# One kernel of attention, experts and gated product: loads, splits and joins around the scan put in other places

## The reference

```python
# 1: a recurrence with complex diagonal decay, gates limited to |a| <= 0.999
for t in range(S):
    new_re = ar * S_re - ai * S_im
    new_im = ar * S_im + ai * S_re
    S_re, S_im = (new_re + kv, new_im)          # kv = outer(k[t], v[t])
    y[:, :, t] = einsum('bhd,bhde->bhe', q[:, :, t], S_re)
# 2: top-1 experts, x = y as (3072, 384)
logits = x @ w_gate + modality_bias[modality_id]
out[mask] = gate_w[mask, None] * (relu(x[mask] @ w1[e]) @ w2[e])
# 3
out = ((x @ mid_w1) * (x @ mid_w2)) @ w3 @ w_out
```

## Time and profile before

| | us |
|---|---|
| median of 3 runs (lowest, highest) | 949.64 (948.28, 953.0) |
| the profiled execution, and its span | 949.64, 947.9 |
| PE busy in it | 798.0 (84%) |
| DVE, ACT, POOL busy | 510.3, 344.2, 128.1 |
| chain that ended last: PE, DVE | 69%, 19% |
| mean granted clock of PE, of full speed | 0.959 |

### The profile page before, as it was taken

How to read it: one execution, slowest core, us unless ns; L and a number is a source line. 1 busy time by engine, 2 the same in 40 slices (tenths; PEclk the granted TensorE clock), 3 DMA queues, 4 the chain that set the end, 5 groups by cost and what they waited for, 6 DMA issues and landing times.

```text
span 947.9 us, 11977 instructions
## 1 busy us (share of the span) xinstructions
PE 798.0 (84%) x4598; PEld 663.3 (70%) x4598; DVE 510.3 (54%) x980; ACT 344.2 (36%) x684; POOL 128.1 (14%) x127
## 2 busy tenths in 40 slices
PE   0039800699999998999999999999999999999995
PEld 0025400388888888778888888878989888888885
DVE  4999999999898855835445445452111121202010
ACT  6921201355545335345245335342222222213120
POOL 0201100000000322200000000002223232323231
PEclk9999955799999998999999999999999999999998
DMA  9981121557666675163433342233000000000000
GB/s 382 378 274 53 59 75 27 142 142 189 173 175 173 174 196 199 52 200 105 132 120 111 104 146 88 67 78 126 25 9 17 17 9 26 9 26 1 34 0 34
DMA packets 49014, 102.95 MB, mean 109 GB/s; under 512 B 12080, under 2 KB 31792, under 8 KB 46640
## 3 DMA queue, kind: packets, MB, share of 16 engines
q1 hardware_dynamic: 43312, 83.11, 28.5%
q0 software_dynamic: 5632, 18.94, 5.7%
HBM read 64.06 MB, written 18.95 MB: 88 GB/s over the span
## 4 chain that ended last, share of the span: by engine, by line
PE 69%; DVE 19%; DMA 3%; SPq 3%; ACT 3%; issue 2%; POOL 0%; DVEq 0%
PE moe_bank L515 18%; PE moe_bank L517 18%; PE moe_bank L516 18%; PE bank L1291 4%; DVE rows L1002 3%; DVE rows L1003 3%; PE bank L1325 2%; DVE gates L1005 2%; PE bank L1341 2%; PE bank L1257 2%; DVE gates L978 2%; DVE gates L1006 2%; SPq L670 1%; DMA gates<-a_im 1%; PE bank L1345 1%
## 5 line engine op out<-in xcount | busy, mean ns | idle before, releaser
L1835 DVE TENSOR_TENSOR u_sb<-x_in,moe_bank 128x512 f32<-128x512 f32 x48 | 33.0, 688 | 229.3 <-PE moe_bank L517 229.3
L1692 POOL TENSOR_TENSOR hid_lo<-u_sb,hid_hi 128x512 fp32r<-128x512 f32 x48 | 62.4, 1300 | 387.8 <-ACT hid_hi L1741 387.8
L517 PE MATMUL moe_bank<-xT_hi,w_lo 128*128 128x512 f32 x288 | 114.1, 396 | 0.0
L515 PE MATMUL moe_bank<-xT_hi,w_hi 128*128 128x512 f32 x288 | 113.7, 395 | 0.0
L516 PE MATMUL moe_bank<-xT_lo,w_hi 128*128 128x512 f32 x288 | 113.3, 394 | 0.0
L1270 PE MATMUL bank<-early_w_out,early_w3T 128*128 128x384 f32 x128 | 45.4, 511 | 66.0 <-DMA early_w_out<-w_out 62.6
L1270 PEld LDWEIGHTS bank<-early_w_out,early_w3T 128*128 128x128 f32 x128 | 24.8, 199 | 85.9 <-issue 64.7
L1756 ACT COPY x_in<-moe_bank 128x512 f32<-128x512 f32 x48 | 28.2, 587 | 149.8 <-PE moe_bank L517 149.8
L515 PE MATMUL moe_bank<-hid_hi,w_hi 128*128 128x512 f32 x168 | 68.0, 405 | 3.9 <-DVE hid_lo L510 2.0
L517 PE MATMUL moe_bank<-hid_hi,w_lo 128*128 128x512 f32 x168 | 67.1, 400 | 0.0
L516 PE MATMUL moe_bank<-hid_lo,w_hi 128*128 128x512 f32 x168 | 67.1, 400 | 0.0
(11 more groups left out here) (196 smaller groups left out, 1698.6 us busy)
## 6 DMA issues: line engine op xcount, KB each, us to landing
stage<-w SPq DMA_DIRECT2D x12, 1536.0 KB, 7.9
ks<-mags SPq DMA_DIRECT2D x48, 144.0 KB, 2.8
x_sorted<-early_zero POOLq DMA_DIRECT2D x8, 772.0 KB, 20.8
qs<-gates SPq DMA_DIRECT2D x40, 146.2 KB
x_in<-x_sorted SPq DMA_DIRECT2D x28, 193.0 KB, 3.7
gates<-a_re SPq DMA_DIRECT2D x4, 1170.0 KB, 12.3
gates<-a_im SPq DMA_DIRECT2D x4, 1170.0 KB, 14.6
spare<-k SPq DMA_DIRECT2D x4, 1152.0 KB, 5.5
```

The costliest lines, as they stand in the source:

```text
L515: nc.tensor.matmul(out, l_hi, r_hi, start=first, stop=False)
L517: return nc.tensor.matmul(out, l_lo, r_hi, start=False, stop=last)
L1692: nc.gpsimd.tensor_tensor(hid_lo[:, f], u_sb[:, f % 2], hid_hi[:, f].bitcast(F32), ALU.subtract).then_inc(u_lo_ready, 1)
L1835: nc.vector.tensor_tensor(u_sb[:, f % 2], a_sb[:, f % 2], bank_b[f % 2][:, :], ALU.mult).then_inc(u_ready, 1)
```

## The change

On SP, the wait for `first_ready` and the two value loads go to the last batch's turn, ahead of `stack_k(3, 1)`, and a W1 piece is issued behind each head's descriptors in it; W2 and x stay where they were. On ACT, W1's splits go from slots 7 and 8 to slots 5, 6 and 7, the scaling of `x_in` comes over from DVE (slots 7, 8, 9), three of W2's splits go into the eight hidden tiles, and the squares of stage 2 go from slot 0 to slot 1 of batch 0. On DVE, `finish(1, 3)` is done before the scan, `join(2, 2)` in slot 0 and `norm(2)` in slot 2; the low halves of W1 and W2 have other slots, W2's tiles 4 to 7 are subtracted by GpSimd behind its last scatter, and the table's parts stand one hidden tile earlier. In step 1 of the experts W1 is split ahead of x, as in the later steps. One wait in the general version is left out.

```diff
--- before.py
+++ after.py
@@ -643,13 +643,13 @@
         n_qs = n_ks + 1
         n_early = 2 * sum(g < -(-HU * D // P) for i in range(HU) for d, n, g, lane in pieces(HU + i))
         RANKS_AFTER = {5 * NCH - 1: 0, 6 * NCH - 1: 1, 7 * NCH - 1: 2}
-        EARLY_W1_HI = {7: (0, 1, 2, 3), 8: (4, 5, 6, 7)}
-        EARLY_W2_HI = {9: (0, 1, 2), 10: (3, 4, 5), 11: (6,)}
-        EARLY_X = {8: (0, 1), 9: (2, 3)}
-        BETWEEN_W1_LO = {8: 0, 9: 3, 10: 6}
-        EARLY_W1_LO = {8: (1, 2), 9: (4, 5), 10: (7,)}
-        BETWEEN_W2_LO = {11: 2}
-        EARLY_W2_LO = {10: (0, 1), 11: (3, 4)}
+        EARLY_W1_HI = {5: (0, 1, 2), 6: (3, 4, 5), 7: (6, 7)}
+        EARLY_W2_HI = {9: (0, 1), 10: (2, 3, 4)}
+        EARLY_X = {7: (0,), 8: (1, 2), 9: (3,)}
+        EARLY_W1_LO = {6: (0, 1), 8: (4, 5), 9: (7,)}
+        EARLY_W2_LO = {10: (1, 2)}
+        BETWEEN_W1_LO = {7: 2, 8: 3, 9: 6}
+        BETWEEN_W2_LO = {10: 0, 11: 3}
...
             return gates[:, x, b * GB:(b + 1) * GB].rearrange("p g (c t) -> p (g c) t", t=PITCH)[:, :, 0:CH]
...
 
-            def stack_k(b, m, planes=((0, seeds), (1, norms))):
+            def stack_k(b, m, first=None, planes=((0, seeds), (1, norms))):
                 for i in range(HU):
                     for d, n, g, lane in pieces(HU * m + i):
                         for c, plane_of in planes:
                             rows = slice(c * D + d, c * D + d + n)
                             sp.dma_start(ks[m][rows, i], plane_of[b][lane:lane + n, g * NCH:(g + 1) * NCH].rearrange(
                                 "p c t -> p (c t)")).then_inc(ks_in[m], DMA)
+                    if first is not None:
+                        load_w1(first, i)
...
                 cols = slice(i * (F // HU), (i + 1) * (F // HU))
...
             stack_q(sp, 0, 1, (RE, IM), range(G1))
             sp.wait_ge(k_half_ready, 1)
-            stack_k(0, 0, ((0, seeds),))
+            stack_k(0, 0, None, ((0, seeds),))
             sp.wait_ge(kt_ready, 1)
-            stack_k(0, 0, ((1, norms),))
+            stack_k(0, 0, None, ((1, norms),))
+            e = None
             for b in range(B):
                 sp.wait_ge(kinv_ready, 2 * b + 2)
                 if b + 1 < B:
                     load_k(b + 1)
                 if b:
                     sp.wait_ge(yT_psum, b * SLOTS)
+                if b == B - 1:
+                    sp.wait_ge(R.first_ready, 1)
+                    e = sp.value_load(L.table[0:1, L.FIRST:L.FIRST + 1], min_val=0, max_val=E - 1)
+                    row = sp.value_load(L.table[0:1, L.ROW0:L.ROW0 + 1], min_val=0, max_val=E * N - BLOCK)
                 sp.wait_ge(kt_ready, 2 * b + 2)
-                stack_k(b, 1)
+                stack_k(b, 1, e)
                 if b:
                     load_v(b, 1)
                 sp.wait_ge(ks_in[1], (b + 1) * (DMA * n_ks))
@@ -754,12 +761,7 @@
                     sp.wait_ge(ks_in[0], (b + 2) * (DMA * n_ks))
                     sp.wait_ge(qt_ready, 2 * b + 2)
                     stack_q(sp, b + 1, 0)
-            sp.wait_ge(R.first_ready, 1)
-            e = sp.value_load(L.table[0:1, L.FIRST:L.FIRST + 1], min_val=0, max_val=E - 1)
-            row = sp.value_load(L.table[0:1, L.ROW0:L.ROW0 + 1], min_val=0, max_val=E * N - BLOCK)
             sp.wait_ge(qs_in[1], B * (DMA * n_qs))
-            for i in range(HU):
-                load_w1(e, i)
             for i in range(HU // 2):
...
             sp.wait_ge(R.sorted_early, L.groups[1][1] * DMA)
@@ -854,7 +856,7 @@
 
...
 
-                if b == 0 and slot == 0:
+                if b == 0 and slot == 1:
                     squares_of(2)
                 if b + 1 < B:
                     if slot == (2 if b == 0 else 1):
@@ -874,13 +876,15 @@
                 if b == B - 1:
                     if slot == 4:
                         route_exp(nc, act, L, R, b - 1)
-                    if slot == 7:
+                    if slot == 5:
                         act.wait_ge(W.w1_first, HU * DMA)
                         act.wait_ge(qt_ready, 2 * B - 1)
                         for i in range(NU):
                             act.wait_ge(ks_in[i], B * (DMA * n_ks))
                     for f in EARLY_W1_HI.get(slot, ()):
                         split_w1_hi(nc, L, L.stage1, f, W.w1_hi_ready)
+                    for q in EARLY_X.get(slot, ()):
+                        scale_x(nc, act, L, W, 0, q)
                     if slot == 9:
                         act.wait_ge(W.w2_first, HU * DMA)
                     for f in EARLY_W2_HI.get(slot, ()):
@@ -928,8 +932,8 @@
             route_exp(nc, act, L, R, B)
             for f in range(KF):
                 hidden_high(nc, act, L, W, bank_scores[f % 2][:, :], 0, f)
-                if f == 0:
-                    split_w2_hi(nc, L, KF - 1, W.w2_hi_ready)
+                if 1 <= f <= 3:
+                    split_w2_hi(nc, L, f + 4, W.w2_hi_ready)
...
             nc.gpsimd.memset(shift[:, 0:1], MAG_EPS)
@@ -952,6 +956,10 @@
                     for loaded in W.x_loaded:
                         pool.wait_ge(loaded, DMA)
                 route_scatter(nc, pool, L, io, R, r)
+            for f in range(4, KF):
+                pool.wait_ge(W.w2_hi_ready, f + 1)
+                nc.gpsimd.tensor_tensor(L.w2_lo[:, f], L.stage2[:, f], L.w2_hi[:, f].bitcast(F32),
+                                        ALU.subtract).then_inc(W.w2_lo_ready, 1)
 
...
             def im_square(b):
@@ -1091,25 +1099,23 @@
                 finish(0, step)
             norm(1)
             join(2, 0)
-            for step in range(3):
+            for step in range(4):
                 finish(1, step)
-            for step in (1, 2):
-                join(2, step)
+            join(2, 1)
 
             def prepare(b, slot):
 
                 now, first, second, after = 2 * b + 1, 2 * b + 2, 2 * b + 3, 2 * b + 4
                 if slot == 0:
-                    if b == 0:
-                        finish(now, 3)
                     finish(now, 4)
                 elif slot == 1:
                     finish(now, 5)
                     finish(now, 6)
                 if b == 0:
-                    if slot == 1:
+                    if slot == 0:
+                        join(first, 2)
+                    elif slot == 2:
                         norm(first)
-                    elif slot == 2:
                         join(second, 0)
                     elif slot == 3:
                         join(second, 1)
@@ -1170,10 +1176,6 @@
                     elif slot == 11:
                         for k in range(2):
                             x_low(nc, dve, L, W, first_xT[k][:, :], 0, k)
-                    for q in EARLY_X.get(slot, ()):
-                        dve.wait_ge(W.x_loaded[q], DMA)
-                        nc.vector.tensor_scalar(L.x_in[:, q, 0:DM], L.x_in[:, q, 0:DM], L.x_in[:, q, DM + 1:DM + 2], None,
-                                                ALU.mult).then_inc(W.x_scaled, 1)
                     for f in EARLY_W1_LO.get(slot, ()):
                         split_w1_lo(nc, dve, L, L.stage1, f, W.w1_hi_ready, f + 1, W.w1_lo_ready)
                     for f in EARLY_W2_LO.get(slot, ()):
@@ -1226,13 +1228,10 @@
             first_low(1)
             V.read_rank(B, last_rank, True)
             V.place(B)
-            for f in (5, 6):
-                split_w2_lo(nc, dve, L, f, W.w2_hi_ready, f + 1, W.w2_lo_ready)
+            V.table_blocks()
             first_low(2)
-            V.table_blocks()
-            split_w2_lo(nc, dve, L, KF - 1, W.w2_hi_ready, KF, W.w2_lo_ready)
+            V.table_steps()
             first_low(3)
-            V.table_steps()
             V.table_pick(slice(0, 2))
             first_low(4)
             V.table_pick(slice(2, 4))
@@ -1550,7 +1549,6 @@
                 V.table_pick(slice(0, 4))
                 V.table_rows()
                 V.table_store()
-                wait_sorted(dve, L, A)
...
             with pe.If(general(pe)):
@@ -1717,12 +1715,9 @@
             def step(j):
                 for q in range(BT):
                     scale_x(nc, act, L, W, j, q)
-                if j > 1:
-                    w1_highs(w1_in, j, w1_hi_ready)
+                w1_highs(w1_in, j, w1_hi_ready)
                 for k in range(KD):
                     x_high(nc, act, L, W, bank_xT[k][:, :], j, k)
-                if j == 1:
-                    w1_highs(w1_in, j, w1_hi_ready)
                 for f in range(KF):
                     hidden_high(nc, act, L, W, bank_hid[f % 2][:, :], j, f)
                     if f == 0:
@@ -1779,14 +1774,11 @@
 
             def step(j):
                 at = dve.value_load(table[0:1, L.OFF + j - 1:L.OFF + j], min_val=0, max_val=N)
-                if j > 1:
-                    w1_lows(j, w1_hi_ready, w1_lo_ready)
+                w1_lows(j, w1_hi_ready, w1_lo_ready)
                 keep(j - 1, at, 0)
                 keep(j - 1, at, 1)
                 for k in range(KD):
```

(2 more changed lines are left out.)

## The result

| | before | after |
|---|---|---|
| first comparison: median of 4 runs (lowest, highest), us | 948.96 (944.96, 953.0) | 962.24 (960.88, 964.29) |
| ratio, 95% interval | | 1.0142 (1.0095 to 1.0190) |
| profiled execution and its span, us | 949.64, 947.9 | 957.92, 956.1 |

The kernel is slower by 1.4%, some 13 us, where 5.5 were forecast; 962.24 lies above the range. The level of both kernels differs between sessions (the median of before was 946 to 963), on one chip too (959.6 and 947.6 on chip 4), so a time is compared only with the kernel before of its own session.

What follows compares the result with a forecast made beforehand. PE hardly waits after the experts' step 0, so scan start, last batch and seam before 430 us decide. 2.9 + 5.3 + 2.4 - 5.1 - 0.9 + 0.9 = +5.5 on 949.64 gave 955.1 us, range 945.5 to 961.

Steps and rivals of the forecast that it cites:

- start of the scan: Batch 0, slots 1 and 2: DVE's new order and later ACT squares delay PE's update of chunk 2, +2.9 us.
- PE before chunk 42: Last batch: W1 loads between stack_k(3, 1)'s descriptors make stack_q(3, 1) late, so PE waits +5.3 us before chunk 42.
- its clock: Behind the wait before chunk 42: TensorE is granted its lower clock for chunks 42 and 43, +2.4 us.
- W1's wait and its clock: Last batch, slot 7: ACT's and PE's wait for W1 and the lower clock behind it go, -5.1 us.
- hot: Seam to the experts: two split_w2_lo leave from ahead of choose(3), so PE's wait for group 3's hot goes, -0.9 us.
- W2's low halves on GpSimd: Seam: GpSimd's subtractions hinder DVE's small table instructions, 2.0, less 1.1 for earlier hidden tile 6: net +0.9 us.
- step 1: Experts, step 1: W1 split ahead of x_high, same instructions in another order, 0 us (bounds 0 and +1.5).
- (a): Rival, last batch: transfers are hidden and chunk 42 starts on time; -2.2, or -4.2 without GpSimd conflict, 945.4 to 947.4; chance 0.17.
- (b): Rival, start of the scan: no loss there, ACT's and DVE's slots 1 and 2 have room; +2.6, 952.2 us; chance 0.13.
- (c): Rival, seam: DVE and GpSimd don't hinder each other where DVE's instructions are small; 953.1 us; chance 0.20.
- (d): Rival, last batch: W1's 1.5 MB delay both stacks by 2 us or more each, x_in late to slot 7; +10, 960; chance 0.12.

Runs made afterwards that it cites:

- e14: The changed kernel unchanged, timed a third time: 962.34 us against 946.47 for the kernel before, ratio 1.0181 (1.0154 to 1.0207).
- e2: Kernel before with only the edits of DVE's first lists and ACT's squares at the start of the scan: ratio 1.0006 (0.9967 to 1.0045).
- e17: Kernel before with only SP's new order (W1 loads between stack_k(3,1)'s descriptors), splits still at slots 7 and 8: 955.69 us, ratio 1.0103 (1.0081 to 1.0125).
- e11: Changed kernel with GpSimd's scatter of group 1 held until the scores of chunk 42: no time given; PE's wait before chunk 42 was 4.94 us.
- e15: Kernel before with W1's loads issued behind v's load, ACT's W1 splits at slots 5 to 7, x scaled by ACT: ratio 1.0060 (1.0041 to 1.0078).
- e16: Kernel before with only W2's low halves 4 to 7 moved to GpSimd: 949.31 us, ratio 1.0027 (1.0011 to 1.0043).
- e10: Kernel before with only step 1's new order: last transposes of step 0 to first hidden matmul 7.74 us, 6.83 before; no whole time given.
- e6: Kernel before with W2's low halves 4 to 7 on GpSimd, spaced apart: first hidden matmul to output(0, 0) 23.44 us, 21.28 before; no whole time given.
- e5: Kernel before, unchanged, run once more for its trace: span 960.8 us.
- e1: The changed kernel unchanged, run again against the kernel before: ratio 1.0080 (1.0044 to 1.0116), 7.7 us slower.
- e3: Kernel before with only SP's new order, W1's splits still at slots 7 and 8: ratio 1.0037 (0.9997 to 1.0077).
- e7: Kernel before with 24 more, shorter matmuls in PE's warm-up, same columns in all: PE's results 5.67 us late at chunk 40; no whole time given.
- e13: Kernel before with W1's loads behind v's, splits at slots 5 to 7, x scaled by ACT, group 1's scatter held until stack_q(3,1) landed: ratio 1.0044 (1.0022 to 1.0066).
- e9: Kernel before with GpSimd's scatter of group 1 held until the scores of chunk 42: late results at chunk 40 gone; no whole time given.
- e18: Kernel before with ACT's W1 splits one slot later (8 and 9), W2's splits and DVE's lists following: ratio 1.0012 (0.9975 to 1.0049).
- e12: Kernel before with GpSimd's scatter of group 1 held until stack_q(3,1) has landed: ratio 1.0047 (1.0022 to 1.0073).
- e4: Kernel before with only W2's low halves 4 to 7 moved to GpSimd: ratio 1.0052 (1.0010 to 1.0094).

## Why the prediction was wrong

Term by term, e14's trace against the trace of before (us):

| step | forecast (bounds) | e14 | others |
|---|---|---|---|
| start of the scan | +2.9 (1.5, 3.3) | +3.0 | 2.6 in e2 |
| PE before chunk 42 | +5.3 (2.7, 9) | +6.35 | 6.9 in e17, 5.1 in e11 |
| its clock | +2.4 (1.2, 3.5) | +5.4 | 4.8 in e17, 4.6 in e15 |
| W1's wait and its clock | -5.1 | -5.1 | -5.1 in e17 |
| hot | -0.9 | -0.9 | |
| W2's low halves on GpSimd | +0.9 (-1.3, 2.5) | +4.2 | 4.3 in e16, 4.6 in after |
| step 1 | 0 (0, 1.5) | +1.2 | 0.9 in e10, 1.7 in after |

e14's scan began 0.7 earlier by itself, and the half clock behind `output(0, 0)` that the first trace of before had (1.57) is not there: 3.0 + 6.35 + 5.4 - 5.1 - 0.9 + 4.2 + 1.2 - 0.7 - 1.6 = 11.9; the spans differ by 11.6. No term had the wrong sign; the sum was 6 too small, most of it in two of them (+3.3 and +3.0). These are differences of single traces.

**GpSimd** is the step that failed first: I let DVE's `hid_lo` and reductions "go on" between the hindered instructions, and counted 2.0 of GpSimd's 3.9 us. But one DVE instruction is held through the whole run of four, and DVE works in order, so all behind it stand: the price is the run, 3.9, and half clock for PE behind a wait of 4.0, less the relief. The Trainium skill, page "SBUF — State Buffer", section "SBUF: two separate sides", says that the port pair is locked for the whole instruction. The traces agree with a lock (0.97 us beside one subtraction in e6), but not with its end after one instruction: 4.62 beside four.

**The clock behind chunk 42** is the second: it was sized by the row of a 2.4 us wait (2.7). After 6.2 and 6.8 us the lower clock was granted before PE resumed and lasted 10 to 12 us from there, 4.8 to 5.4 lost; after 4.1 us, 4.6 lost, and e11's wait of 4.94 us cost 4.6. My upper bound of 3.5 had no row of a wait as long as the one I forecast.

**The wait itself**: in e17 `stack_k` starts 3.3 late (3.55 forecast, against PE's chunks), `stack_q` 6.9 later than that (15.68 instead of 8.82 us, 1.7 forecast), and is issued 2.7 faster without the scatter beside it (2.3 was the bound). The miss is inside: the ten `ks` descriptors and the W1 pieces between them take 2.7 longer to issue, and the last `ks` piece takes 7.36 to land instead of 3.18, W1's traffic beside it. I had +0.3 for all contention. Two errors offset each other in part, so that +5.3 came near 6.35 and 6.9 is partly luck.

**Step 1**: the same instructions do stand between W1's landing and `hidden(1, 0)`, but their order is not free: PE's first hidden tile needs all three `xT_lo` and only the first split. Before, `xT_lo` came first and the splits only had to keep ahead of PE tile by tile; after, it stands behind all eight, and behind two copies that they had pushed back.

**Rivals.** (a), (b), (c) are refuted by the traces of e17, e2 and e16. (d), that W1's bytes hold up the stacks, had the direction: the last piece of `stack_k` took 4.2 longer to land. But `stack_q` wasn't held up and x wasn't late at slot 7 of e14, and that its +10 comes near e14's trace is partly luck, since GpSimd's part of it is none of (d)'s. That the recorded trace of after shows none of the wait at chunk 42 is, I argue, the late results' doing: where before and after both have them (e5 and e1), that wait and the W1 wait are both covered, and the difference is start, GpSimd, step 1 and hot: 2.6 + 4.7 + 1.2 - 0.9 = 7.6 by e1's and e2's traces, against e1's 7.7 (4.2 to 11). That the two agree proves little: e5 had lost 11.1 us to late results and clock by chunk 40 and e1 1.6, and behind chunk 41 the lower clock lasted one chunk in e1 and three in e3 and e7. Which of the first comparison's timed runs had late results can't be shown; the 13.3 there lies between e1's 7.7 and e14's 17.

## What to carry to other kernels

Before a load is put ahead of another on one queue, look for the slack of what stands behind it: here it was 0.27 us, and every way of loading W1 earlier paid at chunk 42 for the wait that it removed, with the clock on top except where the scatter was held back (e13). In this kernel a run of GpSimd instructions held one DVE instruction for the length of the run, so count the run whole; spacing them out won back about half. And one trace is one execution: take a second of both kernels before a term is priced by a row that may not be there the next time.

## What was not expected of the hardware

- PE's results reached ACT and DVE 5.2 to 5.8 us late at chunk 40 in all ten traces of four sessions that had the scatter in its place (e1 to e10 without e9, and e18), and in no trace of two other sessions (e11 to e17, of which e11, e12 and e13 held the scatter back). Chip 4 had a session of each kind (e1 to e4, and e11 to e13). The time of before goes with it: medians of 958.4 to 963.0 in the sessions with five rounds that had them, 946.5 and 947.6 without.
- The clock fell to half within a PE wait of 6.2 us, not behind it. The length of a short wait didn't decide alone: before `output(0, 0)`, 1.02 us in after and 1.88 in e17 left it at full speed, 1.95 in before and 1.80 in e12 did not (0.50 from 414 to 416 us in e12).
